# Banded attention into a routed MLP: scores split by halves of the sequence, keys laid out once per 64 queries, five buffers

## The reference, cut to what matters

```python
# attention: B, H = 4, 8 heads; 512 local positions, 32 global ones; 64 channels a head; window 32
s_g   = scale * q_g @ [k_g, k_l].T            # 32 global queries see all 544 keys
out_g = softmax(s_g) @ [v_g, v_l]
s_ll  = where(abs(i - j) <= 32, scale * q_l @ k_l.T, -1e9)
s_lg  = scale * q_l @ k_g.T                   # each local query also sees the 32 global keys
out_l = softmax([s_lg, s_ll]) @ [v_g, v_l]
x = [out_g, out_l]                            # 4 x 544 rows of 512 channels
# routed MLP: logits = x @ w_gate (8 experts), local gate = x @ w_local; one expert for each row,
# kept from the row before where the gate says so; out = p[e] * relu(x @ w1[e]) @ w2[e]
# then: relu(x @ w_in), a convolution over 3 positions, a sigmoid gate, @ w_out
```

## Time and profile before

| | |
|---|---|
| median of 3 runs | 692.94 us (689.23 to 694.88) |
| the profiled execution | 693.83 us, its span 692.0 us |
| PE busy | 650.1 us, 94% of the span |
| DVE busy | 505.8 us (73%) |
| ACT busy | 355.6 us (51%) |
| POOL busy | 196.6 us (28%) |
| granted TensorE clock, mean | 0.983 of full speed |

### The profile page before, as it was taken

One profiled execution on the slowest core, in us unless ns is written; L12 is line 12 of the kernel. 1 busy time (PEld: TensorE's weight loads), 2 busy tenths in 40 slices (PEclk: granted clock), 3 DMA queues, 4 the chain that ended last, 5 costly groups with the idle time before them and its releaser, 6 DMA issues.

```text
span 692.0 us, 14269 instructions
## 1 busy us (share of the span) xinstructions
PE 650.1 (94%) x4737; PEld 518.5 (75%) x4737; DVE 505.8 (73%) x1001; ACT 355.6 (51%) x567; POOL 196.6 (28%) x160
## 2 busy tenths in 40 slices
PE   3888888899889999999999999998999999999997
PEld 3666666664667888888888888886788888888886
DVE  2665656553858899998989989884489777787772
ACT  2555656541037787877878777783333232321321
POOL 2000000034154555545555555541412020000000
PEclk9999999999889999999999999999999999999999
DMA  8764647238811117163614435400411021100102
GB/s 303 235 212 145 213 143 224 106 123 329 324 62 31 49 44 288 45 239 133 234 45 151 167 114 220 167 16 32 112 41 47 1 91 30 61 0 0 61 1 76
DMA packets 37946, 85.03 MB, mean 123 GB/s; under 512 B 7952, under 2 KB 8976, under 8 KB 37904
## 3 DMA queue, kind: packets, MB, share of 16 engines
q1 hardware_dynamic: 29776, 61.39, 25.8%
q0 software_dynamic: 4960, 17.30, 7.5%
q10 hardware_dynamic: 3168, 5.77, 2.2%
HBM read 69.25 MB, written 15.20 MB: 122 GB/s over the span
## 4 chain that ended last, share of the span: by engine, by line
PE 90%; DVE 5%; DMA 1%; issue 1%; ACT 1%; SPq 1%; POOL 0%; DVEq 0%; POOLq 0%; ACTq 0%
PE ps L858 21%; PE ps L859 21%; PE ps L860 21%; PE ps L699 3%; PE ps L889 3%; PE ps L695 3%; PE ps L669 3%; PE ps L636 2%; PE ps L769 2%; PE ps L672 1%; DVE l_p L1039 1%; PE ps L867 1%; PE ps L637 1%; PE ps L811 1%; PE ps L944 1%
## 5 line engine op out<-in xcount | busy, mean ns | idle before, releaser
L1446 ACT CAST w_h<-slots 128x1024 fp32r x88 | 92.0, 1048 | 46.5 <-issue 23.4
L1452 ACT CAST w_h<-slots 128x1024 fp32r x88 | 89.5, 1050 | 39.2 <-PE ps L860 23.4
L1244 DVE TENSOR_TENSOR w_l<-slots,w_h 128x1024 fp32r<-128x1024 f32 x66 | 88.1, 1384 | 9.9 <-ACT w_h L1446 7.2
L1251 DVE TENSOR_TENSOR w_l<-slots,w_h 128x1024 fp32r<-128x1024 f32 x66 | 77.9, 1233 | 15.7 <-ACT w_h L1452 15.7
L1527 ACT ACTIVATE h_buf<-ps 128x512 f32<-128x512 f32 x32 | 19.2, 601 | 123.8 <-PE ps L860 108.7
L529 POOL TENSOR_TENSOR w_l<-slots,w_h 128x1024 fp32r<-128x1024 f32 x22 | 54.3, 2469 | 72.6 <-ACT w_h L1446 72.6
L858 PE MATMUL ps<-w_h,b_hTh 128*128 128x512 f32 x176 | 71.5, 406 | 2.6 <-DVE b_hTl L1238 2.6
L858 PE MATMUL ps<-w_h,b_xTh 128*128 128x512 f32 x176 | 70.5, 401 | 0.9 <-DVE w_l L1244 0.6
L860 PE MATMUL ps<-w_h,b_hTl 128*128 128x512 f32 x176 | 69.5, 395 | 0.0
L859 PE MATMUL ps<-w_l,b_hTh 128*128 128x512 f32 x176 | 69.3, 394 | 0.0
L860 PE MATMUL ps<-w_h,b_xTl 128*128 128x512 f32 x176 | 68.8, 391 | 0.0
(11 more groups left out here) (230 smaller groups left out, 1394.8 us busy)
## 6 DMA issues: line engine op xcount, KB each, us to landing
slots<-w SPq DMA_DIRECT2D x16, 2048.0 KB, 12.3
l_va<-va SPq DMA_DIRECT2D x16, 520.0 KB, 4.1
l_k<-kw SPq DMA_DIRECT2D x16, 352.0 KB, 3.4
y_sorted<-b_y ACTq DMA_DIRECT2D x22, 256.0 KB, 2.9
l_q<-ql SPq DMA_DIRECT2D x16, 256.0 KB, 3.6
x_rows<-X POOLq DMA_DIRECT2D x4, 1024.0 KB, 5.4
out<-o_l SPq DMA_DIRECT2D x4, 1024.0 KB, 4.3
win<-w_in POOLq DMA_DIRECT2D x1, 2048.0 KB, 12.2
```

What stands on the lines that cost most here:

```text
L1244: vec.tensor_tensor(w_l[:, u, :], unit_of(at, False, u), w_h[:, u, :].bitcast(F32), ALU.subtract).then_inc(w_lo_dve, 1)
L1251: vec.tensor_tensor(w_l[:, u, :], unit_of(at, True, u), w_h[:, u, :].bitcast(F32), ALU.subtract).then_inc(w_lo_dve, 1)
L1446: sca.copy(w_h[:, u, :], unit_of(at, False, u)).then_inc(w_hi, 1)
L1452: sca.copy(w_h[:, u, :], unit_of(at, True, u)).then_inc(w_hi, 1)
```

## The change

The scores of a pair are computed in two halves of the sequence, tiles 0 and 1 and then 2 and 3, instead of all at once. Half 0 of both heads is in banks 0 and 1, half 1 in banks 2 and 3. Each half has its own semaphore counts (`scored`, `maxed`), and PE's, DVE's and ACT's orders are written anew: the two halves of pair 2g+2 are computed at two places of the group, half 1 before turn(2g+1, 1) and half 0 before g_turn(g), and their maxima are taken before normalize(2g+1, 0) and before copy_turned of g.

K is laid out once for each 64 queries, eight times 160 columns instead of four times 160 and 64, with the global keys repeated, so a second block takes one matmul of 160 columns. The narrow one is gone; a pair's K is 640 KB where it was 352 KB. The rings have five buffers. The four small `l_vg` transfers are issued by POOL, with a semaphore of their own; Q of pair 0 and the constants but the masks are issued by ACT at the start; the first K and the masks come first on SP.

In the logits, the four chunks go to four strips of 32 PSUM rows (the gate weights padded to 32 columns), none accumulating on another; the copy takes 128 rows; and `turn_logits` multiplies with a matrix that also adds the four strips, which is an ordinary f32 matmul.

```diff
 VW = DH + 1
-KEYS = NT * TK + HQ
...
-NRING = 6
+NRING = 5
...
-        gate_w = place("const", "gate_w", [P, DC, E + 1])
+        gate_w = place("const", "gate_w", [P, DC, 32])
...
+        def scored(pair, half):
+
+            if pair == 0:
+                return half + 1
+            return 5 * (pair // 2) + (3 + half if pair % 2 == 1 else 2 - half)
+
+        def maxed(pair, half, u):
+
+            if pair == 0:
+                return 2 * half + u + 1
+            return 9 * (pair // 2) + (5 + 2 * half if pair % 2 == 1 else 3 - 2 * half) + u
...
+        def load_queries(eng, pair):
+
+            i = pair % NRING
+            eng.dma_start(l_q[i][:], ql[pair]).then_inc(qk_in[i], 16)
...
         def load_keys(eng, pair):
 
             i = pair % NRING
             eng.dma_start(l_k[i][:, 0:KEYS], kw[pair]).then_inc(qk_in[i], 16)
-            eng.dma_start(l_q[i][:], ql[pair]).then_inc(qk_in[i], 16)
 
         def load_values(eng, pair):
 
             i = pair % NRING
             eng.dma_start(l_va[i][:].rearrange("p x u d -> p (x u d)"), va[pair]).then_inc(v_in[i], 16)
+            eng.dma_start(l_vt[i][:].rearrange("p u d -> p (u d)"), vt[pair]).then_inc(v_in[i], 16)
+
+        def load_blocks(eng, pair):
+
+            i = pair % NRING
             for t in range(NT):
-                eng.dma_start(l_vg[i][SG * t:SG * t + SG, :, t, :], vt[pair, 0:SG].rearrange("p (u d) -> p u d", u=2)
-                              ).then_inc(v_in[i], 16)
-            eng.dma_start(l_vt[i][:].rearrange("p u d -> p (u d)"), vt[pair]).then_inc(v_in[i], 16)
+                eng.dma_start(l_vg[i][SG * t:SG * t + SG, :, t, :], vt[pair, SG:2 * SG].rearrange("p (u d) -> p u d", u=2)
+                              ).then_inc(vg_in[i], 16)
...
         @block.sync
         def _(sp):
             load_keys(sp, 0)
-            sp.dma_start(consts[:], cst).then_inc(const_in, 16)
-            sp.wait_ge(vg_zero, 1)
-            load_values(sp, 0)
-            for pair in range(1, NRING):
-                load_keys(sp, pair)
-                sp.wait_ge(vg_zero, pair + 1)
-                load_values(sp, pair)
+            sp.dma_start(consts[:, C_MASK:NC_CONST], cst[:, C_MASK:NC_CONST]).then_inc(mask_in, 16)
+            for pair in range(NRING):
+                if pair >= 1:
+                    load_keys(sp, pair)
+                    load_queries(sp, pair)
+                if pair >= 1:
+                    load_values(sp, pair - 1)
                 if pair == 1:
                     sp.dma_start(g_q[:], qg).then_inc(gq_in, 16)
+            load_values(sp, NRING - 1)
             sp.dma_start(gate_w[:], wg).then_inc(gate_in, 16)
             sp.dma_start(conv_w[:], cw).then_inc(gate_in, 16)
             for pair in range(NRING, NPAIR):
                 sp.wait_ge(o_ready, sub_g((pair - NRING) // 2) + 1)
                 load_keys(sp, pair)
+                load_queries(sp, pair)
                 load_values(sp, pair)
...
+            for pair in range(NRING):
+                pool.wait_ge(vg_zero, pair + 1)
+                load_blocks(pool, pair)
...
-            for b in range(B - 1):
-                store_batch(b)
+            for pair in range(NRING, NPAIR):
+                pool.wait_ge(o_ready, sub_g((pair - NRING) // 2) + 1)
+                load_blocks(pool, pair)
+                if pair % (H // 2) == 3:
+                    store_batch(pair // (H // 2) - 1)
...
-            def scores(pair):
-
-                i = pair % NRING
+            def scores(pair, half):
...
-                if pair >= 1:
-                    pe.wait_ge(max_ready, sub(pair - 1, 1) + 1)
-                    if pair % 2 == 0:
-                        pe.wait_ge(p_ready, sub_g(pair // 2 - 1) + 1)
-                for t in range(NT):
+                if pair % 2 == 1:
+                    pe.wait_ge(max_ready, maxed(pair - 1, half, 1))
+                elif pair and half == 1:
+                    pe.wait_ge(max_ready, maxed(pair - 1, 1, 1))
+                elif pair:
+                    pe.wait_ge(p_ready, sub_g(pair // 2 - 1) + 1)
+                for t in range(2 * half, 2 * half + 2):
                     at = t % 2 * TK
-                    q = [slice(P * t + HQ * h, P * t + HQ * h + HQ) for h in range(2)]
-                    rows = [slice(DH * u, DH * u + DH) for u in range(2)]
-                    k = l_k[i][:, TK * t:TK * t + TK]
-                    beside = l_k[i][:, TK * t + HQ:TK * t + TK + HQ + SG].rearrange("p (a k) -> p a k", a=2)[:, :, 0:HQ]
-                    for u, r in enumerate(rows):
-                        mm(ps[0:HQ, 2 * u + t // 2, at:at + TK], l_q[i][r, q[0]], k[r], start=True, stop=True)
-                        mm(ps[HQ:P, 2 * u + t // 2, at:at + WK], l_q[i][r, q[1]], beside[r], start=True, stop=True)
-                    for u, r in enumerate(rows):
-                        last = mm(ps[HQ:P, 2 * u + t // 2, at + WK:at + TK], l_q[i][r, q[1]], k[r, WK:TK],
-                                  start=True, stop=True)
+                    q = [slice(P * t + HQ * h, P * t + HQ * h + HQ) for h in two]
+                    rows = [slice(DH * u, DH * u + DH) for u in two]
+                    for u in two:
+                        for h in two:
+                            k_at = TK * (2 * t + h)
+                            last = mm(ps[HQ * h:HQ * h + HQ, 2 * half + u, at:at + TK], l_q[i][rows[u], q[h]],
+                                      l_k[i][rows[u], k_at:k_at + TK], start=True, stop=True)
                 last.then_inc(s_ready, 1)
...
-                pe.wait_ge(max_ready, sub(2 * g + 1, 1) + 1)
+                pe.wait_ge(max_ready, maxed(2 * g + 1, 0, 1))
...
-                    mm(ps[o, 0, P:SL], q, k[:, TK:NT * TK].rearrange("p (t k) -> p t k", k=TK)[:, :, 0:P],
+                    mm(ps[o, 0, P:SL], q, k[:, 2 * TK:NX * TK].rearrange("p (t k) -> p t k", k=2 * TK)[:, :, 0:P],
                        start=True, stop=True)
-                    last = mm(ps[o, 1, 0:2 * SG], q, k[:, NT * TK - SG:NT * TK + SG], start=True, stop=True)
+                    tail = k[:, KEYS - TK + HQ:KEYS + SG].rearrange("p (a k) -> p a k", a=2)[:, :, 0:SG]
+                    last = mm(ps[o, 1, 0:2 * SG], q, tail, start=True, stop=True)
...
-                    pe.wait_ge(v_in[i], 96 * (pair // NRING + 1))
+                    pe.wait_ge(v_in[i], 32 * (pair // NRING + 1))
+                    pe.wait_ge(vg_in[i], 64 * (pair // NRING + 1))
...
-            scores(0)
+            for half in range(2):
+                scores(0, half)
             pe.wait_ge(const_in, 16)
             for g in range(NG):
-                for a in range(2):
-                    if a == 0:
-                        scores(2 * g + 1)
-                    else:
-                        g_scores(g)
-                    turn(2 * g + a, 0)
-                    if a == 1:
-                        weigh(2 * g, 1)
-                    elif g >= 1:
-                        g_weigh(g - 1)
-                    turn(2 * g + a, 1)
-                    weigh(2 * g + a, 0)
+                for half in range(2):
+                    scores(2 * g + 1, half)
+                turn(2 * g, 0)
+                if g >= 1:
+                    g_weigh(g - 1)
+                turn(2 * g, 1)
+                weigh(2 * g, 0)
+
+                g_scores(g)
+                turn(2 * g + 1, 0)
+                weigh(2 * g, 1)
                 if g + 1 < NG:
-                    scores(2 * g + 2)
+                    scores(2 * g + 2, 1)
+                turn(2 * g + 1, 1)
+                weigh(2 * g + 1, 0)
+
+                if g + 1 < NG:
+                    scores(2 * g + 2, 0)
                 g_turn(g)
                 weigh(2 * g + 1, 1)
             g_weigh(NG - 1)
...
-                    last = mm(ps[0:E + 1, 6 + g % 2, 0:n], gate_w[:, c, :], r_xT[g % 2][:, c, 0:n],
-                              start=(c == 0), stop=(c == DC - 1))
+                    last = mm(ps[32 * c:32 * c + 32, 6 + g % 2, 0:n], gate_w[:, c, :], r_xT[g % 2][:, c, 0:n],
+                              start=True, stop=True)
                 last.then_inc(lt_ready, 1)
...
-                    last = nc.tensor.transpose(ps[:, 5, (E + 1) * tile:(E + 1) * (tile + 1)],
-                                               r_lT[:, P * tile:P * tile + P], consts[0:E + 1, C_ID:C_ID + E + 1])
+                    last = mm(ps[:, 5, (E + 1) * tile:(E + 1) * (tile + 1)], r_lT[:, P * tile:P * tile + P],
+                              consts[:, C_SUM:C_SUM + E + 1], start=True, stop=True)
...
-            def negated_max(pair, u):
+            def negated_max(pair, half, u):
 
                 p = l_p[pair % 2][u]
-                dve.wait_ge(s_ready, 3 * (pair // 2) + pair % 2 + 1)
+                dve.wait_ge(s_ready, scored(pair, half))
                 if pair >= 2:
                     dve.wait_ge(t_ready, sub(pair - 2, u) + 1)
-                for t in range(NT):
+                for t in range(2 * half, 2 * half + 2):
```

(96 more changed lines are left out.)

30 lines of the change are left out of this document (15 added, 15 removed).

## The result

The changed kernel takes 666.0 us (median of 4 runs, 664.75 to 667.27), the kernel before, beside it, 693.3 (4 runs, 689.23 to 694.88): 27 us less, a ratio of 0.9615 with a 95% interval of 0.957 to 0.966. The prediction was 663.0, with 654 to 677 as its range. The profiled run of the changed kernel took 667.27, its span is 665.1.

A forecast was written before the change was run, and what follows sets the result against it. PE was taken to bound the kernel, 90% of the last-ending chain. -14.0 + 1.6 - 0.8 - 4.6 - 3.8 - 8.3 = -29.9 gave 663.0 us against the median, range 654 to 677 for 8 in 10.

The forecast's parts named there:

- The wait and the clock: Attention: seven 2.0 us PE waits for DVE's maxima vanish, -14.0; three clock falls vanish, -4.6.
- What is late next: Attention: turn(2g+1, 0) newly waits 0.2 us in each group for ACT's exponentials, +1.6.
- Fewer, wider score matmuls: Attention scores: 32 instructions a pair instead of 48, less one more tail per group; -0.8, between +3 and -4.
- The start: First loads: scores(1) run from 9.4, so the first turn comes 3.8 us earlier; between -5.5 and 0.
- Logits: Logits: four strips side by side and a new turn_logits bring 21.2 us to 12.9, -8.3; bounds -10.1 and +2.5.
- After: Behind the logits: POOL's splitting of `win` still fits, the routing's clock fall may shift; nothing counted.
- The sum: Whole kernel: all terms give -29.9 us, so 663.9 for the profiled execution and 663.0 against the median.
- A: Rival, attention: a late DVE or ACT makes a new wait, 7 to 8 us come back, 671; chance 0.18.
- the strips ran beside each other: Rival, logits: the strips don't run beside each other, +2.5 instead of -8.3, 674; chance 0.06.
- the clock fell in no group: Rival: the clock falls all the same, three falls remain and the routing's comes earlier, 670; chance 0.07.
- PE waited for no K behind the start: Rival, odd pairs' scores from 5 on: the ring of five starves PE of K, 701 and over; chance 0.04.

The follow-up runs named there:

- the experiments with the logits: Two runs: the new logits alone on the kernel before, 690.76 us; the changed kernel with the logits as before, 671.36 us.
- warm_start: Changed kernel plus dummy matmuls on PE, 3 before the first scores and 7 between them and the second: 664.96 us, ratio 0.9598.

## Why the prediction was right, and where its steps were not

**The wait and the clock: right.** It said 7 x 2.0 and three falls away, and that the margin would be 0.45. The trace has 0.54 from the last maximum's end to the scores, of which DVE's signal takes a part. Four memsets delay DVE by 2.0 us and made a wait of 1.66, five delay it by 2.6 and made one of 2.19: so a little under 0.4 was the margin. From the first g_turn to the eighth 17.9 were forecast and 19.3 measured.

**What is late next: right.** The wait of the turn for ACT's exponentials is there, 1.2 us in five, 1.6 in eight had been forecast.

**Fewer, wider score matmuls: direction right, size too small.** A whole pair takes 1.25 us (43.08 to 44.33) instead of 1.48, two halves 0.70 each. That is 0.23 and 0.08 less, 0.3 in a group, where I had 0.1; against K as before the groups show 0.4. (The bounds given, +3 and -4, don't follow from 0 and 0.3 for a pair; those give +1.6 and -3.2.) A second visit to the quadrants costs 2 x 0.70 - 1.25 = 0.15 us. The Trainium skill ("TensorEngine Tiling (Array Packing)", Key Properties) says that a change of tiling mode drains the engine. The trace doesn't contradict it: one more visit costs 0.15, whether a drain makes it or not. At that price it does not decide.

**The start: mis-sized.** -3.8 was forecast, -2.3 measured. Q of pair 1 was issued at 2.21 and landed at 11.14, not at 9.4. The window of that time (columns as in the earlier trace rows):

```profile
2.00:11.14 9.14, 2.41 (x32) 1.78 (x32) 2.65 (x20) 3.96 (x9) 9.14 (x18) 1.00 0.99 356
```

The rate was not lower than I took it (0.34 MB/us): 356 GB/s in 9.14 us are 3.3 MB. But I counted 2.4 MB, as if nothing issued behind Q of pair 1 could move before Q had landed. SP issues `l_va`, `l_vt`, `g_q` and the next pair's K and Q from 2.71 on, POOL its 20 small transfers from 3.14, and some 0.8 MB of all these moved in the same time. Which of them held Q up was not tried. And I carried the gain on to the end: in the profiled run the first group ate it (14.05 us against 11.77), since by the durations its turns and weighs ran at the lower clock. warm_start bears that out: with dummies ahead, the first turn takes 0.66 us and the group 11.5 (12.16 to 23.67).

**Logits: right** (-8.3 forecast, -8.4 measured), in both pieces: strips run nearly four at a time (3.53 / 1.0 = 3.5), and an instruction of turn_logits takes 0.12, as the row with 128-row weights had said. The Trainium skill ("TensorE: Matmul & The Clock Gate", section LDWEIGHTS) says that only the columns of a weight load count. The prediction read from it 0.085 for the new instructions too, and went by the row instead. The loads themselves (PEld; count, busy us, mean ns of one), two groups of before and one of after:

```profile
L755 PEld LDWEIGHTS ps<-consts,X 128*128 128x128 f32 x68 | 7.3, 141 | 1.8 <-issue 1.2 <-DVE r_xT L1118 0.6
L776 PEld LDWEIGHTS ps<-consts,r_lT 9*128 9x128 f32 x17 | 1.4, 135 | 2.9 <-issue 2.8
```

```profile
L821 PEld LDWEIGHTS ps<-consts,r_lT 128*128 128x128 f32 x34 | 4.1, 191 | 2.7 <-issue 2.7
```

The first two are transposes, with 128 rows and with 9: 141 and 135 ns for a load, so the trace agrees with the rule. The third has the form of the first, but is an ordinary f32 product, and its loads take 191. So the step from 0.085 to 0.12 goes with the change from transposes to products and doesn't speak against the rule; no run changes the rows alone.

**After: the step that failed.** "I count nothing" was wrong by 2.1 us in the trace, and the experiments with the logits put the loss at 3 to 4.5. I had looked at POOL and at the clock, not at the DMA. The third expert's load hangs on the splits of `win`, which moved up with attention only, by 19.3 us; the gather hangs on the routing and moved up by 29.1, with the logits too. Their distance shrank from 18 us to 8, and a load of 4 MB was still under way.

**The sum: right in part by cancelling.** By stages of the profiled executions the forecast had -3.7 up to the first g_turn, -17.9 in attention, -8.3 in the logits and nothing behind; measured were 0.0, -19.3, -8.4 and +0.8 (2.1 lost ahead of the experts, 1.3 gained from there on, for which no run has a cause). A start that gave nothing is thus in part made up for by attention.

**Rivals.** No wait took the removed one's place (A), the strips ran beside each other, the clock fell in no group (granted clock 1.00 from 27.62 to 126.21), and PE waited for no K behind the start: with 640 KB each, `l_k` landed in 4.2 us (median, 20 to 130 us; 3.2 in the earlier trace rows). The mechanism of A is real, as the memsets show, but its margin held.

## What to carry to other kernels

Look at the slack of a wait that you remove and at what the clock does behind it: here seven waits of 2 us cost 14 us themselves and 4.6 more by the clock behind three of them. When a change pulls a stage forward, list what else is timed from another event: two chains that move by different amounts can collide on the DMA engines, and a load put behind the small transfer that everyone waits for gave 3.6 us in its stage (4.7 together with the warm clock), though in the total it was clear of the noise only with that other mend.

## What the runs showed of the hardware

- An indirect gather took 3.50 us with no large load beside it (the load held back) and 6.23 beside a load of 4 MB in another queue (the change).
- Seven waits of 1.66 us left the granted clock at 1.00. Of seven waits of 2.00 us, three (before, the loads alone), four (the logits alone) or five (K's layout alone) had a fall behind them, of seven of 2.19 (five memsets) three; what decides a single one is open.
- A weight load of 128 columns of f32 took 141 ns with 128 rows and 135 with 9 for a transpose, and 191 for an ordinary product.
- Eight f32 matmuls of 512 columns took 1.0 us in four strips of 32 columns and 3.53 one after the other.
- From 147.88 to 152.09 in the trace of before PE did nothing but transposes, busy for 3.84 of 4.21 us, and the granted clock was 1.00, as before it.
- Two executions of one kernel (the change, run twice) differed by 2.2 us at the first g_turn, 27.62 and 25.42, with the second turn at 1.09 us in one and 0.63 in the other.
